# The start and the end of a banded attention stage: score banks, distance tables, the first loads and the last weight splits

## What is computed

```python
rel = pos[:, None] - pos[None, :]
is_global = pos[None, :] < int(n_global)
is_local = (rel >= 0) & (rel < int(n_local))
keep = is_global | is_local
dist = np.where(is_global & ~is_local, float(n_local), np.abs(rel))
scores = scale * q @ k.T + (-slopes[:, None, None] * dist)
scores = np.where(keep, scores, -1e9)
a = softmax(scores)            # max subtracted, + 1e-9 in the denominator
x = a @ v
```

```python
u = x + (x.T @ U @ V).T;  u = u + relu(u @ w_ch1) @ w_ch2     # 512 -> 2048 -> 512
k = relu(xk @ w_k);  out = sigmoid(xr @ w_r) * ((k * k) @ w_v)  # 512 -> 1024 -> 512
```

## Time and profile before

| what | value |
|---|---|
| median of 3 runs | 519.31 us (518.36 to 520.0) |
| the profiled execution's own time | 519.39 us |
| its span, first to last instruction | 517.5 us |
| 0 to 5.4 us | TensorE idle: loads, tables, scaling of the first queries |
| 5.4 to 25 us | the first units; TensorE busy 15.64 of 19.60 us |
| 25 to 86.7 us | the rest of attention; TensorE busy 58.51 of 61.70 us |
| 86.7 to 351.1 us | first network; TensorE busy 264.40 of 264.40 us |
| 351.1 to 514.3 us | second network; TensorE busy 163.20 of 163.20 us |
| 514.3 to 517.5 us | the last results and their stores |

### The profile page before, as it was taken

How to read it: one execution, slowest core, us unless ns; L and a number is a source line. 1 busy time by engine, 2 the same in 40 slices (tenths; PEclk the granted TensorE clock), 3 DMA queues, 4 the chain that set the end, 5 groups by cost and what they waited for, 6 DMA issues and landing times.

```text
span 517.5 us, 9413 instructions
## 1 busy us (share of the span) xinstructions
PE 501.8 (97%) x3664; PEld 413.7 (80%) x3664; DVE 184.0 (36%) x480; ACT 130.8 (25%) x352; POOL 242.3 (47%) x234
## 2 busy tenths in 40 slices
PE   3989999999999999999999999999999999999997
PEld 2778887778888888888888888888888888888885
DVE  6776884131322313222131231312443233441223
ACT  3786884111001010010010101121322132212220
POOL 4046667173009000099500829980999579960000
PEclk9998999999999999999999999999999999999999
DMA  6886766004002200025400000000000200020002
GB/s 211 272 285 214 272 201 213 16 6 158 0 1 81 81 0 0 0 82 162 162 0 0 1 0 1 0 0 0 1 0 1 82 0 0 0 81 0 0 0 81
DMA packets 15343, 34.48 MB, mean 67 GB/s; under 512 B 1488, under 2 KB 1872, under 8 KB 15312
## 3 DMA queue, kind: packets, MB, share of 16 engines
q1 hardware_dynamic: 14736, 33.14, 19.0%
q10 hardware_dynamic: 576, 0.92, 0.6%
HBM read 30.91 MB, written 3.15 MB: 66 GB/s over the span
## 4 chain that ended last, share of the span: by engine, by line
PE 94%; DVE 2%; POOL 1%; issue 1%; ACT 0%; DVEq 0%
PE psum L587 25%; PE psum L575 25%; PE psum L640 13%; PE psum L631 13%; PE psum L655 6%; PE psum L426 4%; PE psum L464 2%; PE psum L440 2%; PE psum L472 1%; PE psum L479 1%; PE psum L456 1%; POOL w2l L1094 1%; DVE probs L869 1%; PE psum L487 1%; POOL w2h L1092 0%
## 5 line engine op out<-in xcount | busy, mean ns | idle before, releaser
L977 DVE SCALAR_TENSOR_TENSOR HL<-psum,HH 128x512 fp32r<-128x512 f32 x48 | 33.2, 692 | 173.0 <-ACT HH L767 173.0
L767 ACT ACTIVATE HH<-psum 128x512 fp32r<-128x512 f32 x48 | 28.8, 599 | 230.2 <-PE psum L575 230.2
L575 PE MATMUL psum<-UH,w1h 128*128 (+1 forms) x192 | 74.8, 390 | 0.6 <-POOL w2l L1094 0.6
L587 PE MATMUL psum<-HH,w2h 128*128 128x512 f32 x192 | 75.1, 391 | 0.0
L587 PE MATMUL psum<-HH,w2l 128*128 128x512 f32 x192 | 74.7, 389 | 0.0
L575 PE MATMUL psum<-UH,w1l 128*128 (+1 forms) x192 | 74.7, 389 | 0.0
L587 PE MATMUL psum<-HL,w2h 128*128 128x512 f32 x192 | 74.7, 389 | 0.0
L575 PE MATMUL psum<-UL,w1h 128*128 (+1 forms) x192 | 74.7, 389 | 0.0
L1107 POOL TENSOR_SCALAR w1h<-raw 128x2048 fp32r<-128x2048 f32 x4 | 7.7, 1928 | 118.2 <-PE psum L587 118.2
L1015 DVE TENSOR_TENSOR k_square<-k_relu 128x512 f32<-128x512 f32 x24 | 24.0, 999 | 66.5 <-ACT k_relu L792 66.4
L686 ACT ACTIVATE probs<-probs,neg_max 128x192 f32<-128x192 f32 x96 | 42.5, 444 | 15.3 <-DVE neg_max L869 14.2
(11 more groups left out here) (111 smaller groups left out, 859.3 us busy)
## 6 DMA issues: line engine op xcount, KB each, us to landing
v_in<-in_v SPq DMA_DIRECT2D x16, 384.0 KB, 4.2
raw<-in_moe_w_ch SPq DMA_DIRECT2D x6, 1024.0 KB, 5.0
k_in<-in_k SPq DMA_DIRECT2D x7, 512.0 KB, 4.5
v_rest<-in_v_rest SPq DMA_DIRECT2D x8, 384.0 KB, 3.7
out<-result SPq DMA_DIRECT2D x12, 256.0 KB, 2.0
q_in<-in_q SPq DMA_DIRECT2D x7, 384.0 KB, 3.6
raw<-in_moe_w_ch SPq DMA_DIRECT2D x8, 256.0 KB, 4.5
raw<-in_moe_w_v SPq DMA_DIRECT2D x2, 1024.0 KB, 5.4
```

Source lines behind the costliest of these rows:

```text
L575: mm = pe.matmul(bank[4 + f % 2][:, 0:BLK], w[:, kt, f * P:(f + 1) * P], x[:, kt, ds(blk * BLK, BLK)], start=kt == 0 and n == 0, stop=kt = ...
L587: mm = pe.matmul(bank[d][:, 0:BLK], w[:, f, d * P:(d + 1) * P], x[:, f % 2, :], start=f == 0 and n == 0, stop=f == FQ - 1 and n == 2)
L767: act.activation(HH[:, f % 2, :], bank[4 + f % 2][:, 0:BLK], ACT.Relu).then_inc(hid_high, 1)
L977: dve.scalar_tensor_tensor(out=HL[:, f % 2, :], in0=bank[4 + f % 2][:, 0:BLK], scalar=0.0, in1=HH[:, f % 2, :].bitcast(F32), op0=ALU.max, ...
```

## The change

1. **Score banks.** Units 0, 1 and 2 have pairs of banks of their own: (0, 1), (4, 5) and (6, 7). `scores(1)` and `scores(2)` follow `scores(0)` with no wait for maxima. `scores(3)` waits for `max_done` 4.
2. **Warm-ups.** Eight matmuls of 128x128 zeros stand ahead of `scores(0)` on TensorE; VectorE writes the zeros first.
3. **Distances.** `reaches` works in place in `reach`, without `grid`, with four copies in place of six. The two `glob_far` operations move from VectorE to GpSimd, ahead of the scaling of the first queries. The nine copies are ordered so that after the fifth the table of unit 1's first tile is complete, and its maxima wait for 5 and 9 tile by tile.
4. **Queues.** Pair 0's values are issued by ScalarE right behind its queries and keys. ScalarE scales the second part of pair 0's queries. `U`, `V4` and `mu` go behind pair 1's values.
5. **Pieces.** The last two weight pieces are loaded ahead of pair 7's values, and GpSimd splits the pieces one earlier, the last two between the halves of u.

```diff
+        FIRST_SCORE_BANKS = [(0, 1), SCORE_BANKS, (6, 7)]
...
-                sp.wait_ge(qk_done, UNITS * p + 1)
...
-                load_rest(p)
-                load_main(p, 0)
-                sp.wait_ge(qk_done, UNITS * p + 2)
-                load_main(p, 1)
-                if p == 0:
+                else:
+                    sp.wait_ge(qk_done, UNITS * p)
+                    load_piece(PIECES - 2)
+                    load_piece(PIECES - 1)
+                if p > 0:
+                    sp.wait_ge(qk_done, UNITS * p + 1)
...
+                if p == 1:
                     sp.dma_start(U[:, :, :], mix_u).then_inc(uv_in, 16)
                     sp.dma_start(V4[:, :], mix_v).then_inc(uv_in, 16)
                     sp.dma_start(mu[:, :, :], mus).then_inc(mu_in, 16)
-                else:
+                if 1 <= p < PAIRS - 1:
                     load_piece(p - 1)
-            load_piece(PIECES - 1)
...
-                if n >= 1:
+                if n == UNITS:
+                    pe.wait_ge(max_done, 2 * n - 2)
+                elif n > UNITS:
                     pe.wait_ge(max_done, 2 * n)
...
-                for n in range(1, NU + 3):
-                    if 2 <= n < NU + 2:
+                scores(1)
+                scores(2)
+                for n in range(2, NU + 3):
+                    if n < NU + 2:
                         turn(n - 2)
...
+            pe.wait_ge(zeros_set, 1)
+            for _ in range(WARM_UPS):
+                pe.matmul(bank[MIX_BANKS[0]][:, 0:P], zeros, zeros, start=True, stop=True)
...
+            act.dma_start(v_rest[:, 0, :, :, :, :], vr[0]).then_inc(v_landed[0], 16)
+            for j in range(GROUPS):
+                act.dma_start(v_in[:, 0, j, :, :, :], vm[0][:, j, :, :, :]).then_inc(v_landed[0], 16)
...
+            act.wait_ge(qk_in[0], 32)
+            act.activation(q_in[:, 0, FIRST:S], q_in[:, 0, FIRST:S], ACT.Copy, scale=q_scale[:, 0:1]).then_inc(rest_scaled, 1)
...
-            dve.tensor_scalar(glob_far[:, :], key[:, :], n_global, FAR, ALU.is_ge, ALU.mult).then_inc(dist_step, 1)
...
-            dve.tensor_scalar(glob_far[:, :], glob_far[:, :], n_local, None, ALU.max).then_inc(dist_step, 1)
...
+                        if n == 1 and h == 0:
+                            dve.wait_ge(dist_more, 5 + 4 * i)
...
+            pool.wait_ge(counts_step, 1)
+            pool.tensor_scalar(glob_far[:, :], key[:, :], counts_f[:, 2:3], FAR, ALU.is_ge, ALU.mult).then_inc(glob_step, 1)
...
-                    if p >= 1:
-                        split_u(p - 1, 0)
-                        split_u(p - 1, 1)
+                    for half in range(2):
+                        if p >= 1:
+                            split_u(p - 1, half)
+                        if p == PAIRS - 2:
+                            split_piece(p + half)
                     if 1 <= p < PAIRS - 2:
                         split_piece(p - 1)
-                    elif p == PAIRS - 2:
-                        for k in range(p - 1, PIECES):
-                            split_piece(k)
+                    if p == PAIRS - 3:
+                        split_piece(p)
```

## The result

The changed kernel takes 522.53 us (median of 20 runs, 519.68 to 526.78) against 519.06 us for the kernel before (20 runs on the same chip, 516.43 to 524.23). The ratio is 1.0073, with a 95% interval of 1.0053 to 1.0092. The profiled execution of the changed kernel took 521.57 us (span 519.7, mean granted clock 0.993); that of the kernel before 519.39 (517.5, 0.997). The prediction is wrong in sign.

A forecast was written before the change was run, and what follows sets the result against it. TensorE was taken as the bound, almost always busy from 19.45 us, with removable waits at the start and before the networks. From 519.39 us, minus 2.35 (start), 0 (U and V4) and 0.55 (end), gave 516.5 us, range 512.8 to 518.6.

The forecast's parts named there:

- the other edits cost nothing on the path: Warm-ups in TensorE's 5.4 us idle start, ScalarE's scaling ahead of its first exponential, three further issues: no cost.
- U and V4 at 0 us: First mixing: V4 lands 5.9 us after unit 4's scores start, needed at 5.95; cost 0 us, ends 0 and 3.1.
- rival D: First mixing: V4 takes 7.0 us, TensorE waits 3.1 us and loses 1.7 to the lower clock; 521.3 us, chance 0.07.
- The start: Unit 3's scores start at 13.3 us against 15.66, a gain of 2.35 us; ends 2.7 and 1.2.
- 0.2 if the two engines hold each other up: Unit 0's maxima: low end of their 0.75 us gain, if VectorE and GpSimd exclude each other.
- TensorE's pace: Early scores: TensorE expected slow again at unit 3, 1.55 us per unit's scores, with as much slow work as before.
- W: Rival: TensorE stays fast from the start after the zeros, 1.4 us more gain; 515.1 us, chance 0.19.
- S: Rival: the unexplained 1.7 us stall at unit 10 goes, 3.4 us with its slow clock; 513.1 us, chance 0.16.
- The end of attention: Ahead of the first network: last weight piece ends earlier, removing TensorE's wait; 0.55 us gain, ends 0 and 0.6.
- Sum: Whole kernel: 519.39 - 2.35 - 0 - 0.55 = 516.5 us, chance 0.44.
- L: Rival: loads give the gain back, by late pair 1 keys and a V4 or values wait; 518.5 us, chance 0.14.

The follow-up runs named there:

- e5: Kernel before with 8 matmuls added to TensorE's branch that never runs; 521.99 us, ratio 1.0065 to the kernel before.
- e6: Changed kernel without the mixing loop in TensorE's branch that never runs; 517.33 us, ratio 0.996 to the kernel before.
- e9: Kernel before with only the eight warm-up matmuls added; 523.60 us, ratio 1.0092 to the kernel before.
- e10: Changed kernel without the warm-up matmuls, its other four edits kept; 516.90 us, ratio 0.999 to the kernel before.
- e13: Kernel before with 6 matmuls added to TensorE's branch that never runs; 523.00 us, ratio 1.0062 to the kernel before.
- e1: Changed kernel with U, V4 and mu loaded right behind pair 1's queries and keys; 519.98 us, ratio 1.0027 to the kernel before.
- e14: Changed kernel with U and V4 loaded right behind pair 1's queries and keys, no warm-ups; 515.13 us, ratio 0.992 to the kernel before.
- e12: Changed kernel with U and V4 early, 4 warm-ups, and GpSimd scaling first queries ahead of `glob_far`; 519.61 us, ratio 1.0042 to the kernel before.
- e8: Kernel before with only the change's earlier loading and splitting of weight pieces; 517.60 us, ratio 0.9987 to the kernel before.
- e3: Changed kernel with U and V4 early and the last 1 MB weight chunk held until the network begins; 517.01 us, ratio 0.9978.
- e15: Changed kernel with U and V4 early and 4 warm-ups in place of 8; 519.16 us, ratio 0.9998 to the kernel before.
- e2: Changed kernel with the last 1 MB weight chunk held until the network has begun; 521.44 us, ratio 1.0037 to the kernel before.
- e7: Changed kernel with U and V4 early, last weight chunk held, and 4 warm-ups in place of 8; 516.75 us, ratio 0.9977.
- e16: Changed kernel with U and V4 early, last weight chunk held, and no warm-ups; 514.51 us, ratio 0.9888 to the kernel before.
- e11: Kernel before with U, V4 and mu loaded behind pair 1's values; 519.79 us, ratio 1.0045 to the kernel before.

## Why the prediction was wrong, step by step

- **The step that failed is "the other edits cost nothing on the path: the eight warm-ups lie in the 5.4 us of idle time".** Their time does lie there. Their 32 instructions do not: they move the jump's target across an edge of the instruction stream 84 us later. Price: 2.84 us of wait and 1.55 us of slow clock behind it, 4.4 us in the profiled execution. Shown by e5, e6, e9, e10 and e13.
- **U and V4 at 0 us failed too, by its size.** The issue came at 18.93 us and V4 landed 5.9 us later, not 3.9, so TensorE waited 2.0, and the slow clock made it 2.8. This was rival D's mechanism with a smaller price (3.1 + 1.7 there). I had put two moderate numbers against each other, 5.9 against 5.95, called the difference zero, and kept a chance of 0.07 for what one landing of 7.0 us in the earlier trace rows already spoke of. Shown by e1, and by e14 against e10.
- **The start was right in kind and 0.65 us too large**: unit 3's scores at 13.95, not 13.3. GpSimd's two operations on `glob_far` take 0.60 and 0.72 us, not 0.25 each; both lie beside VectorE's distances. The first queries are ready at 6.67, not 6.0, the maxima at 8.35 in place of 7.65, no earlier than before. The bound "0.2 if the two engines hold each other up" was the right one. What the change did win there is that unit 1 and 2 have banks of their own: exponentials at 10.80 (forecast 10.2, before 12.04). Pair 1's keys landed at 12.1, forecast 12.3. That the collision alone makes these two operations long wasn't tested by a run of its own, but e12 shows a part of it: there the second one runs while VectorE is idle (5.96 to 6.84 us) and takes 0.40 us in place of 0.72, and the first, beside VectorE again, 0.59.
- **TensorE's pace**: slow through unit 3 (1.56 us), as forecast. W did not happen in the changed kernel, and no gain of the warm-ups shows: the scores of its first three units take 4.12 us, as in e10 without them, and e10 (0.999) and e6 with them (0.996) can't be told apart. The pace at the start differs between kernels for a reason that stays open. In e1, which starts with the same warm-ups, the scores of unit 0 take 0.88 us and those of unit 3 1.56; in e14, without warm-ups, those of unit 3 take 0.88 (at 13.62 us), so W's fast unit 3 came without the zeros that W gave as its reason.
- **S**: the wait at unit 10 did go, and another came at 48.70 us with 1.2. These are edges of blocks in attention. They vary from kernel to kernel and cost 0.2 to 2.6 us each; the attention's end lies anywhere from 80.5 to 90.1 us in these traces. I had named the mechanism and then asked of it only whether one wait goes, not where the change puts the others. And it was luck for the forecast of attention's end: behind the first mixing the changed kernel was 2.58 us behind the forecast (28.18 against 27.95 - 2.35 = 25.60), and the next 56.2 us, 58.2 before, gave 1.98 of them back.
- **The end of attention** gave its 0.55 us: no wait for GpSimd, and e8 with this edit alone has 0.9987 (not told apart from no change). Something else was late next.
- **Sum**: forecast 516.5, own time of the profiled execution 521.57, 5.07 more. Attention ends at 84.40 in place of 83.80 (0.60, the 2.58 less the 1.98 above), the wait at the jump 2.84, the slow clock behind it 1.55; the last 0.08 is rounding of spans. Without the jump's wait the changed kernel is e6: 517.33 us. (A slip in the chances: the forecast, W and S with a tenth of L add up to 0.80 for "faster", not 0.79.)

## What to carry to other kernels

An instruction costs its place in the program as well as its time: before pricing added or removed instructions at nothing, look where the engine's blocks of 256 instructions end, above all around a jump, and keep more than 5 us of work between two edges (the longest fetch here was 5.4 us behind the former edge), or little traffic there. The profile's rows of kind "instruction" tell when each block moved. A transfer that is predicted to land just as it is needed is to be priced at the longest landing that the trace shows, not at its own in a quieter stretch. And a small loss that no edit explains is to be tested with code that never runs: it shifts the program and leaves every executed instruction as it was.

## What the runs showed of the hardware that I had not expected

- Code that never runs made a kernel 0.65% slower (e5) and another 1.1% faster (e6, 0.996 against 1.0073).
- A wait "issue" at an edge of a block is 0.2 to 2.6 us in straight code and up to 3.3 us where a jump leaves little work ahead of it. In the table's kernels those of 1.9 us or more are followed by a granted clock of 0.50, for about 3 us or, in e1, e3 and e9, about 7; those of 1.46 us or less are not. The length alone does not decide it: in e10 a wait of 1.46 us for V4 (at 24.43 us) was followed by 0.50 too.
- A transfer of 16 KB with instructions takes 0.9 to 1.5 us at this edge, but starts up to 3.0 us late when a 1 MB load is under way (e15), against -0.1 to 1.2 us with that load held (e2, e3, e7, e16).
- V4's 384 KB landed from 3.8 us (e11) to 6.9 us (e16) after its issue.
- GpSimd's operations on 128x32 took 0.60 and 0.72 us beside VectorE's two operations of 128x384; the second took 0.40 in e12, with VectorE idle.
